# Order of VectorE's work in the odd steps of a fused attention and MLP kernel, and phi of one pair multiplied in two passes

## What is computed

```python
scores = where(causal, -1e9, (q @ k.T) / sqrt(D))      # 4 batches x 8 heads, S = 576, D = 64
local  = softmax(scores) @ v
phi    = where(q > 0, q, exp(q) - 1) + 1
mem    = (phi @ M_prev) / (phi @ z_prev + 1e-6)
x      = g * mem + (1 - g) * local                     # g = sigmoid(beta), per head
x      = (sigmoid(x @ w_gate) * (x @ w_val)) @ w_out   # 2304 tokens, 512 -> 1536 -> 512
out    = (h * clip(h + 3, 0, 6) / 6) @ w_out2          # h = x @ w_in, 512 -> 2048 -> 512
```

## Time and profile before

| | |
|---|---|
| median of 3 runs | 1078.14 us (1076.61 to 1078.37) |
| the profiled execution | 1077.51 us, span 1075.7 us |
| busy: TensorE, its weight loads | 1051.6 us (98%), 985.0 us (92%) |
| busy: VectorE, ScalarE, GpSimd | 710.4 (66%), 639.9 (59%), 539.9 (50%) |
| chain that ended last | TensorE 94%, VectorE 3%, ScalarE 1%, issue 1% |
| mean granted TensorE clock | 0.998 |

### The profile page before, as it was taken

One profiled execution on the slowest core, in us unless ns is written; L12 is line 12 of the kernel. 1 busy time (PEld: TensorE's weight loads), 2 busy tenths in 40 slices (PEclk: granted clock), 3 DMA queues, 4 the chain that ended last, 5 costly groups with the idle time before them and its releaser, 6 DMA issues.

```text
span 1075.7 us, 20584 instructions
## 1 busy us (share of the span) xinstructions
PE 1051.6 (98%) x6736; PEld 985.0 (92%) x6736; DVE 710.4 (66%) x1545; ACT 639.9 (59%) x1438; POOL 539.9 (50%) x558
## 2 busy tenths in 40 slices
PE   5999999999999999999999999999999999999998
PEld 4778999999999999999999999989888988988897
DVE  5997866867867867867835444566677655655553
ACT  5787776777776777776754433465556333544333
POOL 5996657658667668666545563257880101000000
PEclk9999999999999999999999999999999999999999
DMA  8552442542543443443224235255555444454421
GB/s 192 132 143 67 112 117 68 134 111 77 130 112 82 118 114 89 117 115 92 76 65 117 80 98 177 108 166 171 172 187 156 140 116 119 121 172 119 118 58 59
DMA packets 126348, 126.90 MB, mean 118 GB/s; under 512 B 12080, under 2 KB 92464, under 8 KB 126000
## 3 DMA queue, kind: packets, MB, share of 16 engines
q1 hardware_dynamic: 125968, 122.07, 41.1%
q10 hardware_dynamic: 288, 3.67, 0.9%
HBM read 106.30 MB, written 19.40 MB: 117 GB/s over the span
## 4 chain that ended last, share of the span: by engine, by line
PE 94%; DVE 3%; ACT 1%; issue 1%; DMA 0%; SPq 0%; DVEq 0%; ACTq 0%
PE ps L802 88%; PE ps L843 5%; PE ps L856 1%; DVE prob L1540 0%; DMA qk_st<-qk_t 0%; DVE phi L1522 0%; DVE Cb L1733 0%; DVE q_s L1455 0%; DVE Y L1708 0%; ACT h_gate L1318 0%; ACT pt_hi L1138 0%; DVE znorm_e L1512 0%; DVE h_val L1688 0%; DVE znorm L1510 0%; ACT L1318 0%
## 5 line engine op out<-in xcount | busy, mean ns | idle before, releaser
L802 PE MATMUL ps<-x_hi,WG 128*128 128x288 f32 x1536 | 324.8, 297 | 0.3
L802 PEld LDWEIGHTS ps<-x_hi,WG 128*128 128x128 f32 x1536 | 251.6, 188 | 3.1 <-DVE h_val L1688 2.6
L802 PE MATMUL ps<-x_lo,WG 128*128 128x288 f32 x768 | 226.2, 295 | 0.0
L802 PE MATMUL ps<-XC,WC 128*128 128x384 f32 x1008 | 202.5, 336 | 2.1 <-DVE Cb L1733 1.7
L802 PEld LDWEIGHTS ps<-XC,WC 128*128 128x128 f32 x1008 | 180.2, 188 | 17.7 <-issue 3.2
L662 POOL TENSOR_TENSOR WG<-stage,WG 128x512 fp32r<-128x512 f32 x96 | 128.5, 1353 | 98.9 <-ACT WG L1166 98.9
L802 PE MATMUL ps<-wo,G_hi 128*128 128x512 f32 x540 | 168.0, 392 | 0.0
L802 PE MATMUL ps<-h_hi,WO 128*128 128x288 f32 x768 | 165.8, 299 | 0.7 <-DVE Y L1708 0.2
L802 PEld LDWEIGHTS ps<-x_lo,WG 128*128 128x128 f32 x768 | 144.4, 188 | 0.5
L690 POOL TENSOR_SCALAR prob<-prob,rscale 128x128 f32<-128x128 f32 (+4 forms) x160 | 104.0, 668 | 79.8 <-DVE rscale L1500 79.8
L1733 DVE TENSOR_TENSOR Cb<-ps,Cb 128x384 f32<-128x384 f32 x168 | 89.2, 555 | 83.0 <-PE ps L802 81.2
(11 more groups left out here) (136 smaller groups left out, 1939.8 us busy)
## 6 DMA issues: line engine op xcount, KB each, us to landing
WC<-w_in_parts SPq DMA_DIRECT2D x112, 256.0 KB, 2.7
stage<-w_out SPq DMA_DIRECT2D x64, 256.0 KB, 2.9
qk_st<-qk_t SPq DMA_DIRECT2D x54, 288.0 KB, 4.2
stage<-w_gate SPq DMA_DIRECT2D x48, 256.0 KB, 3.7
stage<-w_val SPq DMA_DIRECT2D x48, 256.0 KB, 3.4
w_in_parts<-WC SPq DMA_DIRECT2D x42, 256.0 KB, 2.0
qn_st<-q_n SPq DMA_DIRECT2D x16, 256.0 KB, 3.2
w_in_parts<-WC ACTq DMA_DIRECT2D x2, 1792.0 KB, 7.3
```

What stands on the lines that cost most here:

```text
L802: return pe.matmul(o, l, r, start=start, stop=stop, skip_group_check=True)
```

## The change

- `move_lo` takes a `half`. In step 1, slot 1, the first half of phi 0 (L1478) stays where it was; the second half (L1488) now comes behind the addition of O0 and ahead of that of O1.
- In step 0, slot 4, head 3's low part now comes behind `h_val` of V3 instead of ahead of it.
- For pair 4 alone (`two_passes`), phi is moved whole (128 partitions, one ScalarE and one VectorE instruction for each piece instead of two): `phit[:, 0]` is the high part of both heads and `phit[:, 1]` the low part. `m_hl` is filled for the head's own 64 rows only, the other rows are zeroed by two GpSimd memsets in lead 0, and `times_mem` multiplies twice.
- `times_mem` waits for the low part of head 3 instead of phi 1, and ScalarE waits for the memsets before it fills `m_hl` in lead 4.

```diff
+        def two_passes(n):
+            return isinstance(n, int) and n == FIRST
...
+                if (n, p) == (0, 0):
+                    for j in two:
+                        pool.memset(m_hl[j][:, :].bitcast(F32), 0.0).then_inc(m_zero, 1)
...
             def times_mem(n, odd):
                 pe.wait_ge(m_ready, 2 * (n + 1))
-                pe.wait_ge(lo_done, piece_phi(n, 1) + 1)
+                pe.wait_ge(lo_done, piece_head(n, odd, QT - 2) + 1)
                 pe.wait_ge(x_done, 2 * n + odd)
                 for a, b in ((0, P), (P, S)):
-                    last = mm(head_out(a, b), m_hl[odd][:, :], phit[:, odd, a:b], True, False)
+                    if two_passes(n):
+                        mm(head_out(a, b), m_hl[odd][:, :], phit[:, 0, a:b], True, False)
+                        last = mm(head_out(a, b), m_hl[odd][:, :], phit[:, 1, a:b], False, False)
+                    else:
+                        last = mm(head_out(a, b), m_hl[odd][:, :], phit[:, odd, a:b], True, False)
...
-                    act.activation(phit[own(0), 0, cols], src[own(0), :], ACT.Copy)
-                    dst, src = phit[own(1), 1, cols], src[own(1), :]
+                    if two_passes(n):
+                        dst = phit[:, 0, cols]
+                    else:
+                        act.activation(phit[own(0), 0, cols], src[own(0), :], ACT.Copy)
+                        dst, src = phit[own(1), 1, cols], src[own(1), :]
...
-            def move_lo(n, p, kind, i, r):
+            def move_lo(n, p, kind, i, r, half=-1):
...
-                    dve.tensor_tensor(phit[other(0), 0, cols], src[own(0), :], phit[own(0), 0, cols].bitcast(F32), ALU.subtract)
-                    dst, src, hi = phit[other(1), 1, cols], src[own(1), :], phit[own(1), 1, cols]
+                    if two_passes(n):
+                        dst, hi = phit[:, 1, cols], phit[:, 0, cols]
+                    else:
+                        if half < 1:
+                            dve.tensor_tensor(phit[other(0), 0, cols], src[own(0), :], phit[own(0), 0, cols].bitcast(F32), ALU.subtract)
+                        if half == 0:
+                            return
+                        dst, src, hi = phit[other(1), 1, cols], src[own(1), :], phit[own(1), 1, cols]
...
-                    if (p, i) not in ((0, 3), (0, 4), (1, 4)):
+                    if (p, i) == (1, 1) and turn:
+                        move_lo(n, p, "phi", 0, r, 0)
+                    elif (p, i) not in ((0, 3), (0, 4), (1, 1), (1, 4)):
                         moves(i)
...
                             if g == 0:
                                 moves(i)
-                            else:
+                            if g == 3:
+                                moves(i, slice(1, None))
+                            if g > 0:
                                 hidden_lo(r, g - 1)
-                            if g == 2:
-                                moves(i, slice(1, None))
...
                                 dve.tensor_tensor(y, ps[:, out_bank(j, alone), 0:HALF], y, ALU.add).then_inc(f_y, 1)
+                            if j == 0 and turn:
+                                move_lo(n, p, "phi", 0, r, 1)
```

More of the change, by code:

```diff
@@ L231, in attention_and_mlps @@
         ld_qk, ld_v, ld_phi, ld_m, ld_beta = [sem(x) for x in ("ld_qk", "ld_v", "ld_phi", "ld_m", "ld_beta")]
-        init, v_zero = sem("init"), sem("v_zero")
+        init, m_zero, v_zero = sem("init"), sem("m_zero"), sem("v_zero")
         g_e, g_1, g_r, gates = sem("g_e"), sem("g_1"), sem("g_r"), sem("gates")
@@ L1202, in high_m @@
                 for j in two:
-                    act.activation(m_hl[j][:, own(j)], m_st[:, j, :], ACT.Copy).then_inc(m_hi_done, 1)
+                    rows = own(j) if two_passes(n) else slice(0, P)
+                    act.activation(m_hl[j][rows, own(j)], m_st[rows, j, :], ACT.Copy).then_inc(m_hi_done, 1)
             def x_high(n, p):
@@ L1261, in lead @@
                     move_hi(n, p, "head", 3, None)
+                    act.wait_ge(m_zero, 2)
                     high_m(n)
@@ L1527, in low_m @@
                 for j in two:
-                    dve.tensor_tensor(m_hl[j][:, other(j)], m_st[:, j, :], m_hl[j][:, own(j)].bitcast(F32), ALU.subtract).then_inc(m_ready, 1)
+                    rows = own(j) if two_passes(n) else slice(0, P)
+                    dve.tensor_tensor(m_hl[j][rows, other(j)], m_st[rows, j, :], m_hl[j][rows, own(j)].bitcast(F32), ALU.subtract).then_inc(m_ready, 1)
             def mask_tile(n, p, j):
```

## The result

The changed kernel takes 1082.58 us (median of 6 runs, 1081.71 to 1083.77) against 1077.25 for the kernel before (6 runs, 1075.62 to 1078.37): ratio 1.0051, 95% interval 1.0039 to 1.0064. It is slower, by about 5.3 us. The forecast was 1081.7, range 1073.0 to 1084.0, with slower as the likeliest sign. The profiled executions took 1082.55 and 1077.51 us, with spans of 1080.8 and 1075.7.

The account below looks back on a forecast made before the run. TensorE, busy throughout, bounds the kernel by its starts plus losses between them. -2.1 + 0.6 - 3.1 - 3.3 + 11.5 = +3.6 us on the profiled 1077.51 gives 1081.1, plus 0.63 to the median: 1081.7, range 1073.0 to 1084.0.

Parts of the forecast that it names:

- Part 1: End of lead 4: one phi copy instruction per part shortens TensorE's stop and keeps its clock up; gain 2.1 us.
- Part 2: Pair 4's product with the memory: a second pass for each head, all on TensorE; cost 0.6 us.
- Parts 3 and 4: In the pairs, V5's wait for V3's product and O2's for O0's addition go; gains 3.1 and 3.3 us.
- Part 5: Ahead of O4: `low_q` starts behind GpSimd's L662 and waits, so O2's addition and O4 come late; cost 11.5 us.
- The moved half of phi is held: On VectorE, phi's second half waits until all earlier instructions finish; 0.08 us paid, 0.8 us over ten pairs.
- `low_q` keeps its place: In the pairs, `low_q` still starts first, leaving only 0.41 us a pair: -3.8 us, 1074.3 us; chance 0.25.
- both waits go and nothing follows: In the pairs, VectorE has enough slack before O4: -7.9 us, 1070.2 us; chance 0.05.
- The partial collision: Only the six unlooped pairs collide, at 1.18 us, four lose 0.41: +0.8 us, 1078.9 us; chance 0.10.
- another wait ends the stop in lead 4: Lead 4: the shorter phi copies give nothing while the passes cost; each case 2.1 us higher, no separate chance.

Follow-up runs that it names:

- lowq_early: The changed kernel with `low_q` put ahead of `x_sum` and the phi half; 1069.72 us, ratio 0.9931 to the kernel before.
- v3_only: The kernel before with only the value products put ahead of the copies and the wait in `times_mem` changed; 1080.96 us, ratio 1.0034.
- gate: The changed kernel plus one wait: in the second half-step GpSimd starts the low part of w only after `low_q`; 1074.59 us, ratio 0.9975 to the kernel before.
- before_lowq_later: The kernel before with only `low_q` moved behind the mask of score tile 2; 1085.91 us, ratio 1.0083.

## Why the prediction was right, step by step

- **Part 1** (2.1): 2.4 us up to G0, with the clock at 1.00 as written and a stop of 0.71 us where 0.9 was written. The size leans on the trace of before: the six traces with the old lead take 5.24 to 5.78 us for this stretch, the six with the new one 3.34 to 3.37, so the gain is 1.9 to 2.4. **Part 2** (0.6): as written, 0.64. From the stop to O0 of pair 5 everything together gave 2.1 us, where parts 1 and 2 had 1.5 and V5 of pair 5 another 0.2.
- **Parts 3 and 4** (3.1, 3.3): in the changed kernel both waits are gone. What they were worth is seen where nothing follows: 5.3 us in the ten pairs of lowq_early, 0.6 behind them, and 0.2 for V5 of pair 5 ahead of them, 6.1 against 6.4.
- **Part 5** (11.5): this step decides, and the runs bear it out. In pair 14 `low_q` lasts 1.53 us and O4 begins 7.25 us behind O0 where 7.26 follows from the text. The path has one stop more than written, with the same total: the text has TensorE wait only for Y of O2, and in the trace it first waits for the mask of score tile 2 (0.48 us of a weight load). Measured against the 6.20 of lowq_early, O4 was late by 1.05 us in pairs 8, 9, 12 and 14, by 1.24 in 7, 10 and 13, by 1.37 in 11, and by 0.74 and 0.36 in 5 and 6: 10.4 us, and with 0.10 each for the reload (the next weights could not be loaded ahead) 11.4.
- **The moved half of phi is held**, as weighed in part 5. It starts at 497.45, after the addition ahead of it has ended (497.43), and the next addition starts at 498.18, after it has ended (498.14), while two additions in a row still overlap by 0.10 (0.82 for two). By the Trainium skill ("VectorE: DVE Perf Modes", section "Two Vector instructions with no wait between them") that is what was to be expected, and the trace agrees.
- Two pairs went the other way than written. Pair 10, expected free, collided; pair 6 did not (`low_q` 0.76). Pair 10 cost 1.3 us where 0.3 was written, pair 6 cost 0.5 where 1.4 was. That they nearly cancel, and that 11.4 meets 11.5, is luck. How thin such margins are v3_only shows, where 0.16 us decide.
- **What the sum left out**: the same collision at a second place. In pairs 8 and 12, where x is cut, VectorE's `x_lo` began ahead of GpSimd's before, and begins behind it after. Pair 8, VectorE and GpSimd before, then VectorE, GpSimd and the weight load after:

```profile
252.03 0.98 DVE L1555 TENSOR_TENSOR x_lo<-x_new,x_hi 128x576 fp32r<-128x576 f32 x1
```

```profile
252.34 3.36 POOL L667 TENSOR_TENSOR x_lo<-x_new,x_hi 128x576 fp32r<-128x576 f32 x2
```

```profile
251.73 1.98 DVE L1577 TENSOR_TENSOR x_lo<-x_new,x_hi 128x576 fp32r<-128x576 f32 x1
```

```profile
251.66 3.33 POOL L670 TENSOR_TENSOR x_lo<-x_new,x_hi 128x576 fp32r<-128x576 f32 x2 [0.85 <-ACT x_hi L1188]
```

```profile
255.07 0.19 PEld L808 LDWEIGHTS ps<-h_hi,WO 128*128 128x128 f32 x1 [0.83 <-DVE Y L1732]
```

  GpSimd begins 0.07 us ahead, `x_lo` takes 1.98 us instead of 0.98, and O6 waits 0.83: with the reload 1.9 us for the two pairs. Behind pair 5's output products TensorE lost 0.67 us with the reload to a low part of the head, behind a wait of ScalarE of 3.1 us for a weight transfer, and 0.24 us more ahead of O0 of pair 6. Why is open: lowq_early has the same lead and neither loss, gate has both though its `low_q` is short, and before_lowq_later, which has nothing of the change, has the first of them (3.3 us of ScalarE, 0.75 of the weight load). Together 2.8 us that the prediction did not have.
- So -6.1 + 11.4 + 2.8 = +8.1 us, and 8.1 measured (from G0 to the second MLP +8.66, less 0.64 for the passes, and 0.1 more for the clock), where the text had +5.1. The sum, +3.6, was 2.7 us low against the stages' +6.3, as much as the terms left out. That the forecast time is only 0.9 us off is luck: the stop began 1.2 us earlier in the trace after, and the median before that the forecast started from, 1078.14 of three runs, is 0.9 above that of the six. Between the medians of six lie 5.3 us, against the 3.6 forecast.
- **The rivals.** That `low_q` keeps its place (0.25) is what gate makes true: it measured 1074.6 us where that rival has 1074.3. That both waits go and nothing follows is lowq_early, 1069.7 for 1070.2. What tells these and the forecast apart is which of the two engines' instructions is first. The partial collision (0.10) is the pattern of v3_only, where just the six unlooped pairs with a `low_q` collide; in the changed kernel three of the four looped ones do too. That another wait ends the stop in lead 4 did not come out: the stop fell to 0.71 us.

## What to carry to other kernels

When a change moves VectorE's work against GpSimd's, list the pairs of instructions with SBUF operands on both engines that stand within a few tenths of a microsecond, in every pair and at every place, and ask which starts first: here the order, not the sum of work, set the time. A reordering that looks like a loss can be a gain with one more instruction moved, so look for the new victim before giving it up. A part that is worth nothing alone may be worth its full forecast when what it exposed has been cleared.

## What the runs showed of the hardware

- The law of the collision. Over the traces here a VectorE instruction with both inputs in SBUF that starts while a GpSimd tensor instruction is in flight ends its own data time after that instruction's end: 0.62 us for `low_q` (64x576) in pair 14 of the changed kernel. In the trace of before it is 0.60 to 0.71 us for all 30 `low_q` that began so, 0.30 to 0.38 for 58 `h_lo` (128x288) and 0.61 to 0.62 for 6 `x_lo` (128x576). The one exception in the trace of after is an `h_lo` that began 0.01 us behind GpSimd's instruction, which is as good as together, and took its usual 0.45 us. In v3_only 0.16 us in the relative start turned 0.78 into 1.87 us.
- It is a matter of both operands being in SBUF. In the trace of after, between 100 and 600 us, 43 additions `Y<-ps,Y` that began with a GpSimd tensor instruction in flight took 0.44 to 0.46 us, and so did the 29 that did not; `x_sum` took 0.75 to 0.76 in 22 and 0.76 in the one other. All 20 `low_q` began with one in flight: the 11 that had 0.39 us or more of it ahead took 1.01 to 1.76 us, the 9 that had 0.24 or less took 0.75 to 0.84. That it is a port that the two engines share, and not some other part, no run here separates.
- Whoever comes second pays: in the kernel before GpSimd took 1.83 us in place of 1.30, with slack to cover it. What the change lost in the pairs is for the most part this cost, moved from the engine with slack to the one without.
- The time up to the last matmul ahead of the stop in lead 4 varies by itself: 88.63 to 90.44 us over twelve traces, one of each kernel, in an order that doesn't follow the change's parts. A part worth under 1 us in its end is read better from the distance between two matmuls than from medians.
